# Attention and two MLPs on one core: end tokens zeroed in SBUF, key and query loads apart, weight scaling on VectorE, other steps for transposes and reads, and 48 matmuls ahead of the first scores

## The reference, cut to what matters

```python
# attention: 4 batches x 8 heads, 512 local and 32 global tokens, head size 64
s_g = scale * q_g @ k_all.T;  out_g = softmax(s_g) @ v_all          # global queries see all 544 keys
s_l = concat(scale * q_l @ k_g.T, where(|i-j| <= 32, scale * q_l @ k_l.T, -1e9))
out_l = softmax(s_l) @ v_all                                        # local queries: 32 global keys and a window
x = heads side by side                                              # [4, S, 512], S = 32 + 512
# first MLP, with a layer norm and a residual
xn = (x - mean) / sqrt(var + 1e-6) * g_ln
x = x + relu(xn @ w_ch1) @ w_ch2                                    # 512 -> 2048 -> 512
# second MLP: a convolution over the tokens, with one zero token beyond either end
h = relu(x @ w_in)                                                  # 512 -> 1024
c[s] = sum_k conv_w[k] * h[s + k - 1]
out = (h * sigmoid(c)) @ w_out                                      # 1024 -> 512
```

## Time and profile before

| | us |
|---|---|
| median of 3 runs | 849.16 (848.84 to 849.77) |
| the profiled execution's own time | 854.52 |
| its span in the trace | 852.6 |
| PE busy | 758.1 (89%) |
| DVE, ACT, POOL busy | 408.0, 360.6, 282.1 |

### The profile page before, as it was taken

One profiled execution on the slowest core, in us unless ns is written; L12 is line 12 of the kernel. 1 busy time (PEld: TensorE's weight loads), 2 busy tenths in 40 slices (PEclk: granted clock), 3 DMA queues, 4 the chain that ended last, 5 costly groups with the idle time before them and its releaser, 6 DMA issues.

```text
span 852.6 us, 16634 instructions
## 1 busy us (share of the span) xinstructions
PE 758.1 (89%) x6496; PEld 696.0 (82%) x6496; DVE 408.0 (48%) x990; ACT 360.6 (42%) x917; POOL 282.1 (33%) x241
## 2 busy tenths in 40 slices
PE   2636679998999899989999999999998999999997
PEld 2536568987898788978899988888888999999997
DVE  2536675558555855442111312212227667666664
ACT  3567766755665564344412321111114333333333
POOL 3638664634353342023304232102022222222222
PEclk9968889999999999999999998999999999999999
DMA  7875567445543550135334599561365221211201
GB/s 191 88 161 157 141 184 200 139 137 147 155 116 93 160 154 16 47 117 168 104 104 156 107 117 212 157 164 62 92 160 99 80 80 53 81 58 49 80 9 45
DMA packets 95901, 98.89 MB, mean 116 GB/s; under 512 B 18128, under 2 KB 75600, under 8 KB 95824
## 3 DMA queue, kind: packets, MB, share of 16 engines
q1 hardware_dynamic: 95824, 97.85, 45.3%
HBM read 67.91 MB, written 29.66 MB: 114 GB/s over the span
## 4 chain that ended last, share of the span: by engine, by line
PE 72%; DVE 6%; ACT 6%; DMA 5%; issue 5%; POOL 3%; SPq 2%; ACTq 0%; POOLq 0%; DVEq 0%
PE u_ps L502 30%; PE y_ps L502 21%; PE s_ps L502 14%; PE t_ps L544 4%; PE o_ps L502 4%; DMA xr<-x_rows 2%; DMA kq_raw<-in_kqT 1%; DVE ln_n L809 1%; DMA w_raw<-in_wall 1%; POOL q_st L1075 1%; ACT w_raw L974 1%; DVE bst L794 1%; DVE v_res L715 1%; DMA y_parts<-yT 1%; DVE p_lo L739 1%
## 5 line engine op out<-in xcount | busy, mean ns | idle before, releaser
L816 DVE SCALAR_TENSOR_TENSOR hb<-u_ps,hb 128x384 fp32r<-128x384 f32 (+1 forms) x48 | 28.9, 602 | 178.3 <-ACT hb L988 178.3
L1104 POOL TENSOR_TENSOR hb<-gated,hb 128x272 fp32r<-128x272 f32 x64 | 55.0, 861 | 160.6 <-ACT hb L1016 160.6
L1089 POOL TENSOR_TENSOR w_lo<-w_raw,w_hi 128x1024 fp32r<-128x1024 f32 x24 | 57.1, 2381 | 130.5 <-ACT w_hi L978 130.5
L988 ACT ACTIVATE hb<-u_ps 128x384 fp32r<-128x384 f32 (+1 forms) x48 | 25.3, 527 | 176.4 <-PE u_ps L502 176.4
L502 PE MATMUL u_ps<-xc,w_hi 128*128 128x274 f32 x512 | 99.8, 289 | 0.0
L833 DVE SCALAR_TENSOR_TENSOR conv_h<-relu_h,conv_sb,conv_h 128x272 f32<-128x272 f32 x128 | 88.8, 694 | 4.5
L502 PE MATMUL u_ps<-xn,w_hi 128*128 128x256 f32 x448 | 86.7, 291 | 0.1
L1068 POOL TENSOR_TENSOR k_lo<-kq_raw,k_hi 128x736 fp32r<-128x736 f32 x31 | 56.4, 1820 | 76.4 <-ACT k_hi L898 75.2
L502 PEld LDWEIGHTS u_ps<-xc,w_hi 128*128 128x128 f32 x512 | 80.8, 189 | 0.2
L1002 ACT ACTIVATE relu_h<-u_ps 128x274 f32<-128x274 f32 x64 | 25.6, 400 | 129.2 <-PE u_ps L502 129.1
L502 PE MATMUL o_ps<-v_raw,p_hi 128*128 128x65 bf16 (+1 forms) x384 | 47.4, 201 | 31.0 <-DVE p_lo L739 25.0
(11 more groups left out here) (133 smaller groups left out, 2149.9 us busy)
## 6 DMA issues: line engine op xcount, KB each, us to landing
kq_raw<-in_kqT SPq DMA_DIRECT2D x64, 320.0 KB, 4.7
w_raw<-in_wall SPq DMA_DIRECT2D x24, 512.0 KB, 4.1
xc<-y_parts SPq DMA_DIRECT2D x8, 1096.0 KB, 5.9
v_raw<-in_vx SPq DMA_DIRECT2D x32, 260.0 KB, 5.0
y_parts<-yT SPq DMA_DIRECT2D x16, 512.0 KB, 6.6
xn_parts<-xn SPq DMA_DIRECT2D x14, 512.0 KB, 5.6
xb<-xn_parts SPq DMA_DIRECT2D x14, 512.0 KB, 6.9
y_first<-y_sb SPq DMA_DIRECT2D x17, 256.0 KB, 4.6
```

What stands on the lines that cost most here:

```text
L816: v.scalar_tensor_tensor(out=lo, in0=u_ps[n % 2][:, 0:width], scalar=0.0, in1=hi.bitcast(f32), op0=ALU.max, op1=ALU.subtract).then_inc(hlo ...
L1089: g.tensor_tensor(w_lo[at][:, :], w_raw[j % 2][:, :], w_hi[at][:, :].bitcast(f32), ALU.subtract).then_inc(wlo_ok, 1)
L1104: g.tensor_tensor(hb[sc % HSLOTS][:, 1, 0:CN], gated[sc % 2][:, :], hb[sc % HSLOTS][:, 0, 0:CN].bitcast(f32), ALU.subtract).then_inc(clo_o ...
```

## The change

1. `y_parts` holds only the 544 real tokens. The eight DMAs of zero tokens go; `load_xc` puts 273 tokens in place, and DVE zeroes the one column of each `xc` buffer that stands for the end (`no_token`), once.
2. `kq_raw` becomes `k_raw` and `q_raw`. `load_k` waits for `k_low` of two heads before and stands one step earlier; `load_q` waits as before. Queries of head 0 are loaded first, and constants later, in two semaphores (`mask_in`, `const_in`).
3. The scaling by `g_sb` is one DVE instruction per block (`scale_up`), at the steps of `W_STEP`, which now lie two apart from 13 on; `weights_hi` and `weights_lo` run one step later.
4. `U0` is 23, the norm's transposes are one step later beside their rows (`ln_step`), `PSLOTS` is 4.
5. `x_g` is no longer gathered in SBUF: `store_global` writes to DRAM and `load_xg` reads the tile back at step 68.
6. `load_yl` of the later chunks is at +4 and not +6, `residual` at +5 and not +6; `read_o` is one step earlier.
7. ACT runs one exponent of no use first, and PE 48 matmuls of 128 columns on zeros ahead of the first scores.

```diff
-KSLOTS, QSLOTS, VSLOTS, PSLOTS, HSLOTS = 6, 3, 7, 3, 3
-U0 = 22
+KSLOTS, QSLOTS, VSLOTS, PSLOTS, HSLOTS = 6, 3, 7, 4, 3
+U0 = 23
...
 def ln_step(t):
-    return 72 if t == GT else 16 * (t // QT + 1) + 4 + t % QT
+    return 75 if t == GT else 16 * (t // QT + 1) + 5 + t % QT
...
-W_STEP = [6 + 3 * j for j in range(8)] + [68 + 2 * j for j in range(8)] + [U0 + N1 + 4 + 2 * j for j in range(8)]
+W_STEP = [13 + 2 * j for j in range(8)] + [70 + 2 * j for j in range(8)] + [U0 + N1 + 4 + 2 * j for j in range(8)]
...
-            def load_head(m):
+            def load_k(m):
                 if m == 2:
                     sp.wait_ge(klo0_ok, 1)
+                if m > 2:
+                    sp.wait_ge(klo_ok, m - 2)
+                sp.dma_start(k_raw[m % 2][0:D, :], kqT[m, :, 0:KW]).then_inc(k_in[m % 2], 16)
+                sp.dma_start(k_raw[m % 2][D:P, :], kqT[m, :, 0:KW]).then_inc(k_in[m % 2], 16)
+
+            def load_q(m):
                 if m >= 2:
                     sp.wait_ge(qglo_ok, m - 1)
-                sp.dma_start(kq_raw[m % 2][0:D, :], kqT[m]).then_inc(kq_in[m % 2], 16)
-                sp.dma_start(kq_raw[m % 2][D:P, :], kqT[m]).then_inc(kq_in[m % 2], 16)
+                sp.dma_start(q_raw[m % 2][0:D, :], kqT[m, :, KW:KQW]).then_inc(q_in[m % 2], 16)
+                sp.dma_start(q_raw[m % 2][D:P, :], kqT[m, :, KW:KQW]).then_inc(q_in[m % 2], 16)
...
             def w_load_step(j):
-                return (4 if j < 2 else W_STEP[j - 2] + 1)
+                return 7 if j < 2 else W_STEP[j - 2] + 2
...
-            def store_xg():
+            def load_xg():
+                sp.wait_ge(pv_ok, len(V_SEQ))
                 for r in range(2):
                     sp.wait_ge(xg_out[r], 16 * GH * BATCH)
-                sp.dma_start(x_rows[GT], x_g[:, :]).then_inc(xgs_out, 16)
+                sp.dma_start(x_g[:, :], x_rows[GT]).then_inc(xg_in, 16)
...
-                sp.dma_start(xc[cc % 2][:, :, :].bitcast(f32),
-                             y_parts[b][:, :, CN * c:CN * c + CW]).then_inc(xc_in[cc % 2], 16)
+                sp.dma_start(xc[c][:, :, 1 - c:CW - c].bitcast(f32),
+                             y_parts[b][:, :, (CN - 1) * c:(CN - 1) * c + CN + 1]).then_inc(xc_in[c], 16)
...
-                if s == 4:
-                    sp.wait_ge(const_ok, 1)
-                    zv = eg_sb[:, 2 * SG:P].rearrange("p (b k e) -> p b k e", b=BATCH, k=2 * KT)
-                    for b in range(BATCH):
-                        with nc.allow_non_contiguous_dma(reason="one zero token at each end"):
-                            sp.dma_start(y_parts[b][:, :, 0:1], zv[:, b, :, 0:1]).then_inc(pad_out, 16)
-                            sp.dma_start(y_parts[b][:, :, S + 1:S + 2], zv[:, b, :, 1:2]).then_inc(pad_out, 16)
...
-                    if s == (U0 + N1 + 3 if k == 0 else U0 + N1 + HALF * k + 6):
+                    if s == (U0 + N1 + 3 if k == 0 else U0 + N1 + HALF * k + 4):
                         load_yl(q)
...
-            pe.wait_ge(const_in, 80)
             pe.wait_ge(const_ok, 2)
+            for i in range(48):
+                mm(y_ps[:, 0, 0:P], qg_st[HEADS - 1][:, :], qg_st[HEADS - 1][:, :], True, True)
             for s in range(END):
+                if s == 2:
+                    pe.wait_ge(const_in, 48)
...
+            def scale_up(j):
+                dve.wait_ge(const_in, 48)
+                dve.wait_ge(w_in[j % 2], 16 * (j // 2 + 1))
+                up_part = w_raw[j % 2][:, 0:DM].rearrange("p (k t) -> p k t", k=KT)
+                v.tensor_tensor(up_part, up_part, g_sb[:, :].unsqueeze(2).to_broadcast([P, KT, P]),
+                                ALU.mult).then_inc(wg_ok, 1)
+
+            def no_token(c):
+
+                if c == 0:
+                    dve.wait_ge(up_ok, N1 + HALF)
+                else:
+                    dve.wait_ge(up_ok, N1 + N2)
+                v.memset(xc[c][:, :, c * (CW - 1):c * (CW - 1) + 1].bitcast(f32), 0.0).then_inc(pad_ok, 1)
...
                 if j < 2 * HALF:
-                    for k in range(KT):
-                        last = nc.scalar.mul(raw[:, P * k:P * (k + 1)], raw[:, P * k:P * (k + 1)], g_sb[:, k:k + 1])
-                    last.then_inc(wg_ok, 1)
                     act.wait_ge(wg_ok, j + 1)
...
-                if s > C0 + 3 and (s - C0 - 3) % FT2 == 0:
-                    read_o((s - C0 - 3) // FT2 - 1)
+                if s > C0 + 2 and (s - C0 - 2) % FT2 == 0:
+                    read_o((s - C0 - 2) // FT2 - 1)
```

More of the change, by code:

```diff
@@ L189, in attention_mlp @@
         x_loc = [sb(xs, f"x_loc{r}", [P, QT, DM]) for r in range(2)]
-        x_g = sb(xs, "x_g", [P, DM])
         ln_n = [sb(xs, f"ln_n{r}", [P, DM]) for r in range(2)]
@@ L197, in attention_mlp @@
         a = ExitStack()
-        kq_raw = [sb(a, f"kq_raw{r}", [P, KQW]) for r in range(2)]
+        k_raw = [sb(a, f"k_raw{r}", [P, KW]) for r in range(2)]
+        q_raw = [sb(a, f"q_raw{r}", [P, S]) for r in range(2)]
         k_hi = [sb(a, f"k_hi{r}", [P, KW], f32r) for r in range(KSLOTS)]
@@ L226, in attention_mlp @@
         xb[0] = sb(x2, "xb0", [P, 2 * KT, 512], f32r)
+        x_g = sb(x2, "x_g", [P, DM])
         x2.close()
@@ L254, in g_ps @@
             return y_ps if G < 2 else s_ps
-        const_in, const_ok, mask_ok = sem("const_in"), sem("const_ok"), sem("mask_ok")
-        kq_in = [sem(f"kq_in{r}") for r in range(2)]
+        mask_in, const_in, const_ok, mask_ok = sem("mask_in"), sem("const_in"), sem("const_ok"), sem("mask_ok")
+        warm_ok = sem("warm_ok")
+        k_in = [sem(f"k_in{r}") for r in range(2)]
+        q_in = [sem(f"q_in{r}") for r in range(2)]
         v_in = [sem(f"v_in{r}") for r in range(VSLOTS)]
@@ L356, in store_global @@
                 for h in range(GH):
-                    sp.dma_start(x_g[SG * b:SG * (b + 1), (r * GH + h) * D:(r * GH + h + 1) * D],
+                    sp.dma_start(x_rows[GT, SG * b:SG * (b + 1), (r * GH + h) * D:(r * GH + h + 1) * D],
                                  x_glo[SG * h:SG * (h + 1), :]).then_inc(xg_out[r], 16)
@@ L441, in store_out @@
                 sp.dma_start(outT[b][:, :, CN * c:CN * (c + 1)], y_sb[:, :, :]).then_inc(out_out, 16)
-            load_head(0)
+            load_q(0)
+            load_k(0)
+            for u in range(2):
+                sp.dma_start(mask_raw[u], maskp[:, u, :]).then_inc(mask_in, 16)
+            load_k(1)
+            load_q(1)
             sp.dma_start(identf[:, :], ident).then_inc(const_in, 16)
-            for u in range(2):
-                sp.dma_start(mask_raw[u], maskp[:, u, :]).then_inc(const_in, 16)
+            for m in range(3):
+                load_v(m)
             sp.dma_start(g_sb[:, :], gln).then_inc(const_in, 16)
             sp.dma_start(conv_sb[:, :, :], convw).then_inc(const_in, 16)
-            load_head(1)
-            for m in range(3):
-                load_v(m)
             for s in range(END):
                 for m in range(2, NHEADS):
+                    if max(2 * m - 7, 0) == s:
+                        load_k(m)
                     if max(2 * m - 6, 0) == s:
-                        load_head(m)
-                if s == 4:
-                    sp.wait_ge(const_ok, 1)
-                    zv = eg_sb[:, 2 * SG:P].rearrange("p (b k e) -> p b k e", b=BATCH, k=2 * KT)
-                    for b in range(BATCH):
-                        with nc.allow_non_contiguous_dma(reason="one zero token at each end"):
-                            sp.dma_start(y_parts[b][:, :, 0:1], zv[:, b, :, 0:1]).then_inc(pad_out, 16)
-                            sp.dma_start(y_parts[b][:, :, S + 1:S + 2], zv[:, b, :, 1:2]).then_inc(pad_out, 16)
+                        load_q(m)
                 for m in range(3, NHEADS):
@@ L650, in up_c @@
                     pe.wait_ge(xc_in[cc % 2], 16 * (cc // 2 + 1))
+                    if cc < 2:
+                        pe.wait_ge(pad_ok, cc + 1)
                 if sc < FT2:
@@ L784, in ln_sums @@
                 if b == BATCH:
-                    for r in range(2):
-                        dve.wait_ge(xg_out[r], 16 * GH * BATCH)
+                    dve.wait_ge(xg_in, 16)
                     rows = [x_g[:, :]]
@@ L888, in _ @@
                     ln_sums(s // 16 - 1)
-                if s == 71:
+                if s == 72:
                     ln_sums(BATCH)
+                if s in W_AT and W_AT[s] < 2 * HALF:
+                    scale_up(W_AT[s])
+                if s == U0 + N1 + HALF + 2:
+                    no_token(0)
+                if s == C0 + 1:
+                    no_token(1)
         @block.scalar
@@ L1023, in read_o @@
                     nc.scalar.copy(y_sb[:, m, :], yb[m][:, 0:CN]).then_inc(oe_ok, 1)
+            act.wait_ge(const_ok, 1)
+            nc.scalar.activation(nbias[:, 0, 0:1], minus_half[:, 0:1], ACT.Exp).then_inc(warm_ok, 1)
             act.wait_ge(const_ok, 2)
-            act.wait_ge(const_in, 80)
-            for m in range(2):
-                k_high(m)
-                q_high(m)
```

(4 more changed lines are left out.)

63 lines of the change are left out of this document (30 added, 33 removed).

## The result

The changed kernel takes 795.77 us (median of 4, 795.03 to 797.87) against 849.46 for the kernel before on the same chip: a ratio of 0.937, 95% interval 0.9349 to 0.9391, or 53.7 us less. The prediction said 803.4 with 790 to 822. The profiled execution has a span of 793.7 us against 852.6, 58.9 less, and took 795.49.

A forecast was written before the change was run, and what follows sets the result against it. PE was taken as the bound from 116 us on, late steps before it. Terms −23.9 (first scores included), −2.5, −6, −3 and −10.4 summed to −45.8: median 849.2 to 803.4 us, 80% between 790 and 822.

The forecast's parts named there:

- First scores: Kernel start: first scores move from 12.91 to 9.7 us, −3.2 us (−0.6 to −4), counted within the start's −23.9.
- The term of the 48 matmuls: Kernel start: 48 matmuls on zeros take 5 to 10 us from about 2 us, ending between 7 and 12.3.
- Steps 8 to 23: Attention steps ahead of the MLP: 61 us, so step 23 starts at 91.7 us, −23.9 (−33.6 to −13.6).
- rival 1: The start stays slow: step 23 at 102 us, norm gives 1, reads nothing; −27.5, 821.7 us; chance 0.22.
- The number 1.28: Steps 8 to 23: assumed ratio of time taken to POOL's 47.4 us of work, chosen between 1.1 and 1.42.
- One step less beside the MLP: 54 to 116 us: step 22 now runs ahead of U0 instead of along with a unit, −2.5 us.
- Norm: Norm's transposes one step behind DVE's rows, so PE's 9.0 us of waits shrink: −6 us (0 to −9).
- Scaling on DVE: 16 weight-block scalings, near 0.69 us each, eight in the steps to 28, lie in DVE's idle time: 0 us.
- Reads: Later chunks, around 492 to 518 us: load_yl ahead of SP's weight load, about 3.5 us earlier, −3 (0 to −3.6).
- Copies: Conv chunk ends: ACT's four copies run during the next chunk's up_c, all seven PE waits go, −10.4 (−9.5 to −10.4).
- Rival 3: Slower: each of 16 DVE scalings stalls with POOL, 0.69 us plus a 2.26 wait, 47 us; 850.6; chance 0.03.
- Rival 2: All goes well: factor 1.1, norm −9, reads −3.6, together −59.1 us, 790 us; chance 0.11.

The follow-up runs named there:

- e1: The changed kernel without the 48 matmuls on zeros; first scores 4.4 us sooner, step 23 at 90.82 us; its total time isn't given.
- e2: The kernel before with the zero tokens alone changed (no DMAs of zeros, y_parts of S columns, DVE clears); 17.4 us faster than the kernel before by medians.
- e9: The kernel before with zero tokens changed and the first eight weight blocks at steps 13, 15, ... 27; 5.6 us more gain than e2 by the ratios.
- e8: The changed kernel with the first eight weight blocks back at steps 6, 9, ... 27; 9.1 us slower than the changed kernel by medians.
- e3: The changed kernel with the scaling of w_up back on ACT, four instructions per block; median 4.7 us above that of e1.
- e4: The changed kernel with the four batches' norm transposes and rows one step earlier, at their old steps; median 4.7 us above that of e1.
- e12: The changed kernel with each head's key loads held back to its queries' step and wait; median 0.8 us above the changed kernel's.
- e11: The changed kernel with the first eight weight blocks later still, scaled in steps 18 to 28; step 23 at 90.28 us, total time not given.
- e6: The changed kernel with the second norm's row reads and POOL's residual sums back at their old steps; 797.16 us against 796.81 for the changed kernel.
- e7: The changed kernel with y_parts S + 2 columns wide again, tokens from column 1, still no zero DMAs; 10.0 us slower than the changed kernel by medians.

## Why the prediction was right, and where it was not

**First scores, 9.7 us.** Measured 12.51. The term of the 48 matmuls was mis-sized: I took the middle of 5 and 10 us between two paces, and the slower one held to the end. That the pace would halve in the scores ("about half of the 0.21 us") was wrong as well. "TensorE: Matmul & The Clock Gate" of the Trainium skill, Part 1, by which they would begin at half and end at full clock in some 7.3 us, is not borne out by this trace, the 7.3 us being the prediction's estimate from it: 10.3 us, all at one pace. Neither had consequences, since step 2 waits for POOL's queries of the second head and for the last constant (e1); step 8 starts at 31.17 where the working had 30.7.

**Steps 8 to 23, 61 us, and step 23 at 91.7.** Measured 58.7 and 89.91. The term was right in size (−25.7 for −23.9) and its cause wrong in part. The step that failed is the one that put the time down to the zero tokens, "The 20.3 us between steps 8 and 9 are the largest part of it". This gap did give most, 16.3 us, but without the zero DMAs alone 7.6 us of it stayed, and unit 0 came 11.0 us sooner of 26.0. The stall of 14.27 us was real and went; ACT's and DVE's queues filled part of it. The weight steps, which I had counted against the change in rival 1, are for it: 2.5 us alone, 12.8 undone. Scaling, norm and the coupled loads add 1.6, 2.6 and 2.2 by undoing, little over the scatter of 2. These don't add up to 26.0 by parts done alone (13.5).

The steps show where it lies. Step 8 starts 3.7 us sooner (31.17 against 34.84), and zero tokens alone leave it at 35.31, so that is the new order of the first loads or another part of the start. Then come the 16.3 us between steps 8 and 9. From the start of step 9 to that of step 22 it is 50.1 us and not 60.5, and one more step ahead of the MLP takes 4.7 back. In the experiments the stretch from step 9 to step 22 is 61.7 us in e2, 63.4 in e9, 60.8 in e8, but 50.2 in e3, 51.5 in e4 and 52.3 in e12. So the late weight steps are needed for these 10 us, and aren't enough for them; what else is needed stays open. The fourth buffer for the exponents (`PSLOTS`), the order of the first loads, `U0` and the place of `weights_hi` and `weights_lo` were undone in no experiment.

The number 1.28 was an interpolation on POOL's work, and its count is off by a block: the earlier trace rows have four `w_lo` for steps 9 to 22, not five, and the changed kernel has four from step 8 to 23. By four, the old factor is 60.5 / 40.3 = 1.50 and the measured one 58.7 / 45.1 = 1.30. Whether POOL's total sets this pace isn't settled: e11 took 4.7 us from it, gained 2.0 by step 22 and lost them to a late weight load.

**One step less beside the MLP, −2.5.** Not tried alone. It has its place in units 40 to 56, where the gain is 7.4 us: e4 explains 3.5, e3 0.5, and the rest, 3 to 4, is left for this and for the row of `x_g` (1.06 us of idle time before, none after), which no experiment separates.

**Norm, −6 (0 to −9).** Undone, 7.1 in the trace, 5.6 without the 1.5 that precede the norm, and 4.7 in the times. PE's waits at the norm's transposes went from some 15 to 10.4 us. The warning that p_lo would take the rows' place held for 4.4 and 2.0 us in the first three batches. What the prediction didn't see is that the last batch, with no attention beside it, gives half of the gain.

**Scaling on DVE, 0.** Wrong by 3.4 to 5.0 us on the good side (with or without the 1.6 at unit 0). The working counted what it costs DVE, not what it takes from ACT, though ACT has 47.48 of 62 us busy in the earlier trace rows and stands in the chain between two PE steps.

**Reads, −3.** The trace gained 5.8 at this place, so the term was near by luck: its mechanism is refuted (e6: nothing). The step "With `load_yl` ahead of that weight load, about 3.5 us earlier, most goes" read the wait of the earlier trace rows from the order of SP's issues. The queue was slow for another reason, the stores into `y_parts`, four of which took 14.6 us to land, and no row of the prediction has them. The change removed them by making the rows of `y_parts` S wide, which the prediction counted as part of the zero tokens and priced at nothing. e2 alone has the 5.8 us.

**Copies, −10.4.** Right in mechanism, 12.1 in the trace (seven times 1.73): each chunk end also lost 0.24 us beside its 1.49 of idle time.

**Rivals.** Rival 3 was refuted for this kernel: one scaling of 16 shows its long form, and a second took 1.55 us. Rival 1's start did not come; its step 23 at 102 us doesn't follow from its own factor either, since 1.42 times 47.4 is 67.3 and gives 98. Rival 2's start came in part: the trace's 58.9 us is near its 59.1, but by other terms, which is luck. Against my 45.8 the trace has 2.8 more at the stores, 5.0 for the scaling (1.6 of it in the start, where it can be scatter), 1.7 at the copies, up to 1 at the norm, 1.0 early in the conv stage (also in e2, so the rows of `y_parts`), and 0.2 to 1.8 at the start. The medians show 53.7, since the kernel before was profiled in an execution of 854.5 and runs at 849.5.

None of the kernels beats the changed one by more than its runs scatter; e1 shows that 48 matmuls can be left out at no loss.

## What to carry to other kernels

Where a queue is late, look up the landing time of each transfer ahead in it before blaming the order: rows of 2,184 bytes with their tokens 4 bytes in, in place of rows of 2,176, made plain stores 1.7 to 2.9 times slower (e7 against the changed kernel), and what was queued behind them late. When work moves from one engine to another, count what leaves the first as well as what the second takes, and ask whether the instruction will now wait for its DMA in front of work that others need. Starting PE earlier is worth nothing while the inputs of a step soon after, here POOL's queries and the last constant, come at a fixed time. Where a trace names a DMA as releaser, look up when it landed before calling another engine the cause.
